# Sliding-window attention inside a fused MLP kernel: two steps at a time, score halves folded into one of 64 keys, a wide softmax over three engines

## The chip, the cores and the metric

One core of a Trainium2 chip runs the kernel. The metric is the device time of one execution in microseconds, as the median of several runs. The core has TensorE (matmul, and the weight loads that precede each), VectorE, ScalarE, GpSimd and SyncE, each with a queue of its own that is worked through in order; semaphores join them. SyncE only issues DMAs.

## The reference, cut to what matters

```python
batch, n_heads, seq, head_dim = (4, 8, 576, 64)
scores = (1 / sqrt(64)) * q @ k.T
mask = (rel >= 0) & (rel < 64)          # rel = query position - key position
scores = where(mask, scores, -1e9)
scores = scores - max(scores)
attn = exp(scores)
attn = attn / (sum(attn) + 1e-9)
x = attn @ v                            # 2304 tokens x 512
h = (x @ w1) * (x @ w2) @ w3 @ w_out    # 512 -> 1024 -> 1024 -> 512
y = x' @ w_in; y = max(0.01 * y, y); y @ w_out2   # 512 -> 2048 -> 512
```

All is float32. The window is 64 keys wide, and queries are taken in blocks of 64, so a block sees two blocks of keys: its own, up to and with the diagonal, and the one before it, above the diagonal. For each query row exactly one of the two halves holds a valid key at a given place, so every row has at most 64 valid keys.

## The kernel before

**Stages.** The products are three passes over high and low parts of float32r (lines 406 to 408), in a seven-product scheme on blocks of 384 tokens. The stages are: the product of the two small weight matrices in 16 slots of 12 matmuls of 512 columns (`wprod_slot`, the early stage); the products of x with w1 and w2 in 168 slots of 6 matmuls of 384 columns (`ab_product`, the order of `AB_SEQ`); and then the later products, which have no part in the change. Attention is laid between the slots of the first two: the first third of it into the early stage, the rest into the second.

**Attention before.** There are 36 steps, each a block of 64 queries of one sequence with all 8 heads, 9 steps to a sequence. Steps go in pairs for the scores and the values. `scores(g)` makes 8 matmuls of 64x64 with 128 keys moving (64 for a step that opens a sequence) into PSUM, two heads on the partitions and four on the free axis. On VectorE `mask_scores` scales and adds the mask in one pass from PSUM to SBUF (L1228) and takes the negated max (L1233). On ScalarE `exps` runs four Exps of 128 columns, each with a bias and an accumulated sum (L841). VectorE adds epsilon and inverts (L1239, L1243), GpSimd multiplies (`normalize`, L771). TensorE turns the 128x128 blocks, four transposes a step (`turn`, L1690), ScalarE copies the turned blocks from PSUM (`turn_copy`, L835), and `values(g)` makes 8 matmuls with 128 rows contracted (L1680). ScalarE or, in the early stage, VectorE copies the values out (`values_copy`, L851, L1248).

**Order.** All is placed by hand, by slots of TensorE. In the early stage the scores of pair p stand behind slot 2p, the turns behind slots 2p+2 and 2p+3, the values behind slot 2p+4. In the second stage the scores stand at slot S (5, 11, 17, 23, 29, 35, 62, 68, 74, 80, 86, 92), the turns in the middle of slots S+8 and S+11, the values at S+12. Each engine runs one loop over the same slots, in which softmax work stands among other work:

- VectorE, early stage, iteration k: values copy, mask passes of what was scored in slot k-1, half of a weight "fill" where `P0_LO` says so (`split_fill`, L1196), the low parts of the pieces for slot k+1 (`split_piece`, L1184), then the sums. Slot k+1 of TensorE waits for these pieces.
- ScalarE: `turn_copy`, the high parts of the pieces, the Exps, fills, and in iteration 7 the copies of two finished banks (`save_wsum`), for which slot 8 waits.
- GpSimd: `normalize`, and the sums of weight quarters (`fill_sums`, four instructions, in iterations 1, 4, 8 and 11 and four times in the second stage; `presums` later).
- In the second stage VectorE makes the sums and products of the seven-product scheme, for which later slots wait with about two slots of slack, and half fills in rounds 1 and 2.

Of the kernel before, what the change touches and what calls it, by code (L numbers as in the profile page):

```python
# [5 lines left out]
F32 = mybir.dt.float32  # L6
F32R = mybir.dt.float32r
ALU = mybir.AluOpType
# [3 lines left out]
P = 128  # L12
# [30 lines left out]
YR0 = AR  # L43
# [32 lines left out]
SCORES0 = tuple(range(CSTEPS))  # L76
TURN0, VALUES0 = 2, 3
SCORES = {}
for _c in range(2):
    for _j in range(CSTEPS):  # L80
        SCORES[(_c + 1) * CSTEPS + _j] = slot_of(4 * _c, 5 + 3 * _j)
EXPS_A, EXPS_B, RECIP, TURN, VALUES = 2, 3, 4, 8, 9


SCORED, VALUED = {}, {}
for _g in range(NSTEP):
    SCORED[_g] = SCORES0[_g - _g % 2] if _g < CSTEPS else SCORES[_g - _g % 2]
    VALUED[_g] = SCORES0[_g | 1] + VALUES0 if _g < CSTEPS else SCORES[_g | 1] + VALUES
# [12 lines left out]
def width(g):  # L101
    return KW if g % NB else BQ
# [113 lines left out]
def build(nc, qk_steps, v_steps, masks, w3, wo, w12, w_in, w_out, out):  # L216
    with ExitStack() as ctx:
# [32 lines left out]
        negmax = sb("negmax", 2 * HP)  # L250
        sums = sb("sums", 2 * HP)
        sums_eps = sb("sums_eps", 2 * HP)
        rsum = sb("rsum", 2 * HP)
# [5 lines left out]
        mask_s = at(2048, 2 * KW).rearrange("p (b k) -> p b k", b=2)  # L259
        v_raw = at(2304, 2 * DM).rearrange("p (r n) -> p r n", r=2)  # L260
        pt = [at(n, HP * P) for n in (3328, 3840, 1536, 4352)]
        probs = [p.rearrange("p (h k) -> p h k", h=HP) for p in pt]
# [31 lines left out]
        ps_more = ctx.enter_context(nc.psum_tensor("ps_more", [P, 512], F32))  # L294
        ps_v = ctx.enter_context(nc.psum_tensor("ps_values", [P, 512], F32))
        ps_turned = ps_more[:, :].rearrange("p (h k) -> p h k", h=HP)
        ps_heads = ps_v[:, :].rearrange("p (h b q) -> p h b q", h=HP, b=2)
# [9 lines left out]
        probs_zero = sem("probs_zero")  # L307
# [5 lines left out]
        masked = sem("masked")  # L313
        max_done = sem("max_done")
        exp_done = sem("exp_done")
        eps_done = sem("eps_done")
# [3 lines left out]
        pt_done = sem("pt_done")  # L320
# [179 lines left out]
        def _(sp):  # L500
# [70 lines left out]
            def load_qk(g):  # L571
                if g >= 2:
                    sp.wait_ge(scores_done, g - 1)
                sp.dma_start(qk[:, g % 2], qk_steps[g]).then_inc(qk_in[g % 2], 16)

            def load_v(g):
                if g >= 2:
                    sp.wait_ge(values_done, g - 1)
                sp.dma_start(v_raw[:, g % 2], v_steps[g]).then_inc(v_in[g % 2], 16)
# [20 lines left out]
            def load_ty(k):  # L600
                if k == 0:
                    sp.wait_ge(values_done, NSTEP)
                    sp.wait_ge(xs_lo, NPROD * NC2)
# [57 lines left out]
            for k in range(WSLOTS):  # L661
                for i in pieces_for(k + 2) if k else ():
                    load_piece(i)
                for g in range(2, CSTEPS + 2):
                    if SCORED[g - 2] == k - 1:
                        load_qk(g)
                    if VALUED[g - 2] == k - 1:
                        load_v(g)
# [11 lines left out]
            for n in range(NSEQ):  # L680
                r = AB_SEQ[n][0]
                m = n - slot_of(r, 0)
                for g in range(CSTEPS + 2, NSTEP):
                    if SCORED[g - 2] == n - 1:
                        load_qk(g)
                    if VALUED[g - 2] == n - 1:
                        load_v(g)
                if r > 0 and m == (4 if slot_of(r, 3) in VALUED.values() else 3):
                    store_p(r - 1)
                    store_p_late(r - 1)  # L690
# [70 lines left out]
        def _(pool):  # L761
# [5 lines left out]
            def normalize(g):  # L767
                r = g % 2
                pool.wait_ge(rsum_done, g + 1)
                w = width(g)  # L770
                pool.tensor_tensor(probs[g % 4][:, :, 0:w], probs[g % 4][:, :, 0:w],  # L771
                                   rsum[:, r * HP:(r + 1) * HP].unsqueeze(2).to_broadcast([P, HP, w]),
                                   ALU.mult).then_inc(probs_done, 1)
# [21 lines left out]
            for k in range(WSLOTS):  # L795
                for g in range(CSTEPS):
                    if SCORES0[g] == k - 1:
                        normalize(g)
                if k in P0_SUMS:
                    fill_sums(P0_SUMS[k])  # L800
            for n in range(NSEQ):
                for g in range(CSTEPS, NSTEP):
                    if SCORES[g] + RECIP == n:
                        normalize(g)
# [8 lines left out]
        def _(act):  # L813
# [19 lines left out]
            def turn_copy(g):  # L833
                act.wait_ge(turned, g + 1)
                act.activation(probs[g % 4], ps_turned, ACT.Copy).then_inc(pt_done, 1)  # L835

            def exps(g, pairs):
                r, w = g % 2, width(g)
                act.wait_ge(max_done, g + 1)
                for u in pairs:  # L840
                    act.activation(probs[g % 4][:, u, 0:w], probs[g % 4][:, u, 0:w], ACT.Exp,  # L841
                                   bias=negmax[:, r * HP + u:r * HP + u + 1], scale=1.0,
                                   accum_out=sums[:, r * HP + u:r * HP + u + 1]).then_inc(exp_done, 1)

            def values_copy(g):
                q, j = g // CSTEPS, g % CSTEPS
                act.wait_ge(values_done, g + 2)
                if j == 0:
                    act.wait_ge(xs_lo, NPROD * q)
                t0 = j % (CSTEPS // 2) * BQ  # L850
# [1105 lines left out]
```

## Time and profile before

| | |
|---|---|
| median of 3 runs | 732.0 us (731.67 to 732.21) |
| span of the profiled execution | 728.8 us |
| TensorE matmul busy | 722.2 us, 99% of the span, 5032 instructions |
| VectorE busy | 530.9 us, 73% |
| ScalarE busy | 416.7 us, 57% |
| GpSimd busy | 101.8 us, 14% |
| granted TensorE clock | 1.000 |
| DMA | 181.13 MB, mean 249 GB/s |

The profiled execution has no time of its own beside its span; the runs lie 2.9 to 3.4 us above it, 3.2 for the median. A busy share near 99% for TensorE says that matmuls follow each other, since their lengths overlap: what counts is the step from one start to the next. In the rows, a start and a length stand first (us), and "idle before" gives what ended a wait.

### The profile page before, as it was taken

The numbers are of one execution on the slowest core, as the hardware profiler recorded it, in microseconds if no ns is written. First come the engines' busy times: TensorE is split into PE (matmuls) and PEld (weight loads), VectorE is DVE, ScalarE is ACT, GpSimd is POOL, SyncE is SP. The second block draws the span as 40 slices with busy tenths as digits, with TensorE's granted clock in tenths as the row PEclk, the third lists the DMA queues.
The fourth block names the chain that finished last, engine by engine and source line by source line (L and its number), as shares of the span: only waits on it lengthen the run. The fifth ranks groups of instructions, "written<-read, shape, count | busy, mean of one in ns | idle before, by whom it ended". The sixth has DMA issues, their size and how long they took to land.

```text
span 728.8 us, 13804 instructions
## 1 busy us (share of the span) xinstructions
PE 722.2 (99%) x5032; PEld 697.9 (96%) x5032; DVE 530.9 (73%) x834; ACT 416.7 (57%) x888; POOL 101.8 (14%) x122
## 2 busy tenths in 40 slices
PE   9999999999999999999999999999999999999998
PEld 7788989999999999999999999999999999999998
DVE  6988888797767679798668968569788655445552
ACT  5876677646664345665555655456677534544541
POOL 3433474413333120000000000000000000000000
PEclk9999999999999999999999999999999999999999
DMA  9884667655754689989857998987996468778773
GB/s 340 291 293 164 206 232 232 200 163 164 244 175 160 195 291 389 324 279 322 289 193 279 318 298 285 364 278 247 381 370 240 128 186 239 206 212 236 208 199 119
DMA packets 96835, 181.13 MB, mean 249 GB/s; under 512 B 7936, under 2 KB 55680, under 8 KB 96768
## 3 DMA queue, kind: packets, MB, share of 16 engines
q1 hardware_dynamic: 90032, 166.62, 69.1%
q10 hardware_dynamic: 6736, 13.63, 5.1%
q8 instruction: 40, 0.66, 0.4%
q14 instruction: 27, 0.22, 0.1%
HBM read 111.80 MB, written 68.42 MB: 247 GB/s over the span
## 4 chain that ended last, share of the span: by engine, by line
PE 61%; DVE 0%; issue 0%; ACT 0%; DVEq 0%
PE acc L406 10%; PE acc L408 9%; PE acc L407 9%; PE ps_pair L406 5%; PE ps_pair L408 5%; PE ps_pair L407 5%; PE ps_more L408 3%; PE ps_values L408 3%; PE ps_more L406 3%; PE ps_values L406 3%; PE ps_more L407 3%; PE ps_values L407 3%; DVE weights_b L1196 0%; DVE arena L1377 0%; DVE arena L1382 0%
## 5 line engine op out<-in xcount | busy, mean ns | idle before, releaser
L406 PE MATMUL acc<-parts,weights_a 128*128 128x384 f32 (+1 forms) x320 | 112.2, 351 | 0.1
L408 PE MATMUL acc<-parts,weights_a 128*128 128x384 f32 (+1 forms) x320 | 109.5, 342 | 0.0
L407 PE MATMUL acc<-parts,weights_a 128*128 128x384 f32 (+1 forms) x320 | 109.3, 341 | 0.0
L406 PE MATMUL acc<-parts,weights_b 128*128 128x384 f32 x320 | 109.1, 341 | 0.2 <-ACT arena L899 0.2
L408 PE MATMUL acc<-parts,weights_b 128*128 128x384 f32 x320 | 107.1, 335 | 0.0
L407 PE MATMUL acc<-parts,weights_b 128*128 128x384 f32 x320 | 107.0, 334 | 0.0
L1462 DVE TENSOR_TENSOR parts<-raw_c,parts 128x768 fp32r<-128x768 f32 x64 | 61.1, 958 | 61.6 <-ACT parts L958 61.5
L958 ACT ACTIVATE parts<-raw_c 128x768 fp32r<-128x768 f32 x64 | 54.0, 846 | 68.9 <-DMA raw_c<-g_between 66.4
L406 PEld LDWEIGHTS acc<-parts,weights_a 128*128 128x128 f32 x320 | 60.1, 188 | 4.6 <-issue 1.7
L841 ACT ACTIVATE arena<-arena,negmax 128x128 f32<-128x128 f32 (+1 forms) x144 | 55.2, 386 | 15.4 <-DVE negmax L1233 15.3
L406 PEld LDWEIGHTS acc<-parts,weights_b 128*128 128x128 f32 x320 | 60.1, 188 | 1.7 <-issue 0.7
L408 PEld LDWEIGHTS acc<-parts,weights_a 128*128 128x128 f32 x320 | 60.1, 188 | 1.7
L407 PEld LDWEIGHTS acc<-parts,weights_a 128*128 128x128 f32 x320 | 60.2, 188 | 1.4
L407 PEld LDWEIGHTS acc<-parts,weights_b 128*128 128x128 f32 x320 | 60.1, 188 | 0.0
L408 PEld LDWEIGHTS acc<-parts,weights_b 128*128 128x128 f32 x320 | 60.1, 188 | 0.0
L937 ACT ACTIVATE arena<-arena 128x384 f32<-128x384 f32 x72 | 35.9, 524 | 41.0 <-DVE arena L1331 18.7
L771 POOL TENSOR_TENSOR arena<-arena,rsum 128x512 f32<-128x512 f32 (+1 forms) x36 | 40.9, 1137 | 100.7 <-DVE rsum L1243 100.7
L912 ACT ACTIVATE parts<-arena 128x768 fp32r<-128x768 f32 x42 | 35.3, 848 | 34.1 <-PE ps_pair L408 10.6
L1403 DVE TENSOR_TENSOR parts<-arena,parts 128x768 fp32r<-128x768 f32 x42 | 39.5, 953 | 13.7 <-ACT parts L912 13.6
L1331 DVE TENSOR_TENSOR arena<-acc,arena 128x384 f32<-128x384 f32 x60 | 31.7, 552 | 17.6 <-PE acc L408 13.1
L406 PE MATMUL ps_pair<-parts,weights_b 128*128 128x384 f32 x120 | 40.2, 335 | 0.0
L407 PE MATMUL ps_pair<-parts,weights_b 128*128 128x384 f32 x120 | 40.1, 334 | 0.0
(213 smaller groups left out, 1764.2 us busy)
## 6 DMA issues: line engine op xcount, KB each, us to landing
g_between<-arena SPq DMA_DIRECT2D x75, 384.0 KB, 4.8
raw_c<-g_between SPq DMA_DIRECT2D x64, 384.0 KB, 3.5
arena<-p_between SPq DMA_DIRECT2D x42, 384.0 KB, 5.2
arena<-qk_steps SPq DMA_DIRECT2D x36, 384.0 KB, 5.0
arena<-v_steps SPq DMA_DIRECT2D x36, 256.0 KB, 3.7
p_between<-arena SPq DMA_DIRECT2D x24, 384.0 KB, 5.9
x_between<-arena ACTq DMA_DIRECT2D x21, 384.0 KB, 5.4
arena<-x_between SPq DMA_DIRECT2D x21, 384.0 KB, 5.2
```

What stands on the lines that cost most here:

```text
L406: eng.matmul(out_ap, w_hi, m_hi, start=start, stop=False, skip_group_check=resumed)
L407: eng.matmul(out_ap, w_hi, m_lo, start=False, stop=False, skip_group_check=resumed)
L408: return eng.matmul(out_ap, w_lo, m_hi, start=False, stop=stop, skip_group_check=resumed)
L771: pool.tensor_tensor(probs[g % 4][:, :, 0:w], probs[g % 4][:, :, 0:w], rsum[:, r * HP:(r + 1) * HP].unsqueeze(2).to_broadcast([P, HP, w]), ...
L841: act.activation(probs[g % 4][:, u, 0:w], probs[g % 4][:, u, 0:w], ACT.Exp, bias=negmax[:, r * HP + u:r * HP + u + 1], scale=1.0, accum_ou ...
L912: act.activation(block_places[k % NPROD][:, 0:BW], ty_raw[TY_SLOT[k]], ACT.Copy).then_inc(ty_hi, 1)
L937: act.activation(g, g, ACT.Prelu, alpha=SLOPE).then_inc(g_done[q], 1)
L958: act.activation(block_places[k % NPROD][:, 0:BW].rearrange("p (j t) -> p j t", j=2), t_source(k), ACT.Copy).then_inc(t_hi, 1)
L1331: dve.tensor_tensor(dest, bank(r, i, s)[:, 0:CT], p1_sb[:, s], ALU.add).then_inc(c11_done, 1)
L1403: dve.tensor_tensor(b[:, BW:2 * BW], ty_raw[TY_SLOT[k]], b[:, 0:BW].bitcast(F32), ALU.subtract).then_inc(ty_lo, 1)
L1462: dve.tensor_tensor(lo, t_source(k), hi.bitcast(F32), ALU.subtract).then_inc(t_lo, 1)
```

## The change

A pair of steps becomes the unit everywhere (18 "duos" in place of 36 steps). The scores stay as they are, except that an opening step writes its own keys to the upper half of its place.

- ScalarE copies the own-keys half of all 16 blocks from PSUM to SBUF (`fold_copy`), 512 columns.
- VectorE overwrites it under a mask with the half of the keys before (`copy_predicated`, once, or twice where a step of the pair opens a sequence), then takes the max over 64 keys, 8 results a partition.
- GpSimd adds the negated max (`shift`); ScalarE runs one Exp of 512 columns with the scale of 1/8 in it; VectorE sums (`tensor_reduce`), adds epsilon, inverts; GpSimd multiplies as before.
- TensorE turns the pair with 4 transposes in place of 8 (`turn`, at 2p+3 and at S+10).
- VectorE writes two masked copies of the turned block from PSUM (`unfold`), one for the keys before and one for the own keys, in place of ScalarE's two copies.
- `values` makes 32 matmuls of 64 rows and 64 columns, two accumulating into each place, in place of 16 of 128 rows; an opening step needs half as many. The results go to two banks.
- The sums and the inversion move one iteration later in the early stage (k-2 for k-1) and to S+5 from S+4 and S+7; the Exps go to S+3, the shift to S+2.

```diff
+            def shift(p):
+                r = p % 2
+                pool.wait_ge(max_done, p + 1)
+                pool.tensor_tensor(probs_flat[r], probs_flat[r],
+                                   negmax[:, r * H:(r + 1) * H].unsqueeze(2).to_broadcast([P, H, BQ]),
+                                   ALU.add).then_inc(shifted, 1)
...
             for k in range(WSLOTS):
...
+                for p in range(CPAIRS):
+                    if SCORED[p] == k - 1:
+                        shift(p)
+                    if SCORED[p] == k - 2:
+                        normalize(p)
                 if k in P0_SUMS:
                     fill_sums(P0_SUMS[k])
...
+            def fold_copy(p):
+                act.wait_ge(scores_done, p + 1)
+                if p >= 2:
+                    act.wait_ge(turned, p - 1)
+                act.activation(probs[p % 2], ps_own, ACT.Copy).then_inc(fold_copied, 1)
+
+            def exps(p):
+                act.wait_ge(shifted, p + 1)
+                act.activation(probs_flat[p % 2], probs_flat[p % 2], ACT.Exp, scale=float(D) ** -0.5).then_inc(exp_done, 1)
...
+            def fold(p):
+                r = p % 2
+                dve.wait_ge(fold_copied, p + 1)
...
+                if whole:
+                    dve.copy_predicated(probs[r], earlier.unsqueeze(1).unsqueeze(1).to_broadcast([P, 2, HP, BQ]),
+                                        ps_before).then_inc(folded, 2)
...
+                dve.tensor_reduce(negmax[:, rr], probs_flat[r], AX.X, ALU.max, negate=True).then_inc(max_done, 1)
+
+            def invert_sums(p):
+                rr = slice(p % 2 * H, (p % 2 + 1) * H)
+                dve.wait_ge(exp_done, p + 1)
+                dve.tensor_reduce(sums[:, rr], probs_flat[p % 2], AX.X, ALU.add).then_inc(sums_done, 1)
...
+            def unfold(p):
+                dve.wait_ge(turned, p + 1)
+                if p > 0:
+                    dve.wait_ge(values_done, p)
+                for c in range(2):
+                    dve.tensor_tensor(pt[c].rearrange("p (u q) -> p u q", q=BQ), ps_more.rearrange("p (u q) -> p u q", q=BQ),
+                                      mask_s[:, 1 + c].unsqueeze(1).to_broadcast([P, H, BQ]), ALU.mult).then_inc(unfolded, 1)
...
+            def values(p):
+                for b in range(2):
+                    pe.wait_ge(v_in[b], 16 * (p + 1))
+                pe.wait_ge(unfolded, 2 * p + 2)
+                pe.wait_ge(x_done, 2 * p)
+                for b in range(2):
+                    for t in range(2):
+                        for c in range(2):
+                            if c == 0 and opens(2 * p + b):
+                                continue
+                            for r in range(2):
+                                for a in range(2):
+                                    d, rows = slice(a * D, (a + 1) * D), slice(r * BQ, (r + 1) * BQ)
+                                    turned_at = ((b * 2 + t) * 2 + (a ^ t)) * BQ
+                                    last = pe.matmul(ps_heads[r][d, t, b], v_raw[rows, b, c, t, a],
+                                                     pt[c][rows, turned_at:turned_at + BQ],
+                                                     start=c == 0 or opens(2 * p + b), stop=c == 1)
+                last.then_inc(values_done, 1)
+
+            def turn(p):
+                pe.wait_ge(probs_done, p + 1)
+                pe.wait_ge(x_done, 2 * p)
+                for n in range(4):
+                    last = pe.transpose(ps_more[:, n * P:(n + 1) * P], probs[p % 2][:, n // 2, n % 2 * 2:n % 2 * 2 + 2], ident[:, :])
+                last.then_inc(turned, 1)
```

## Rows read from the trace of the kernel before

**Rows 1.** The page's busy line: us, share of the span, instructions.
```profile
PE 722.2 (99%) x5032; PEld 697.9 (96%) x5032; DVE 530.9 (73%) x834; ACT 416.7 (57%) x888; POOL 101.8 (14%) x122
```

**Rows 2.** TensorE's waits: us in total, times, longest.
```profile
PE ps_more L1690 <- POOL arena L771: 1.5, 1, 1.5
```

**Rows 3.** Windows: length, busy us of each engine (x instructions), clock, DMA.
```profile
5.00:70.00 65.00, 64.82 (x628) 52.03 (x628) 54.89 (x93) 48.04 (x145) 26.01 (x28) 1.00 0.78 276
76.00:108.00 32.00, 30.33 (x333) 28.16 (x333) 27.49 (x48) 21.87 (x71) 21.56 (x21) 1.00 0.66 216
```

**Rows 4.** Timeline of TensorE around one turn: start, length, instruction.
```profile
86.38 0.60 PE L1690 MATMUL ps_more<-ident,arena 128*128 128x128 f32 x4
86.73 0.42 PE L406 MATMUL acc<-weights_a 128*128 128x384 f32 x1
86.99 0.34 PE L407 MATMUL acc<-weights_a 128*128 128x384 f32 x1
87.16 0.34 PE L408 MATMUL acc<-weights_a 128*128 128x384 f32 x1
```

**Rows 5.** TensorE: values of a pair, then 64-wide scores; lengths of scores (ns).
```profile
103.44 1.15 PE L1680 MATMUL ps_values<-arena 128*64 128x64 f32 x32
...
104.52 0.46 PE L1700 MATMUL ps_pair<-arena 64*64 64x64 f32 x16
...
L1700 PE MATMUL ps_pair<-arena x576: 216/269/321, 8.3 to 203.6; 64*64 64x128 f32 x168, 64*64 64x64 f32 x24
```

**Rows 6.** Softmax instructions by form: count, busy us, mean ns, idle before.
```profile
L1233 DVE TENSOR_REDUCE negmax<-arena 128x4 f32<-128x512 f32 x32 | 22.0, 686 | 1.1
L1228 DVE SCALAR_TENSOR_TENSOR arena<-ps_pair,arena 128x512 f32<-128x512 f32 x32 | 21.7, 679 | 0.9 <-PE ps_pair L1700 0.7
L1239 DVE TENSOR_SCALAR sums_eps<-sums 128x4 f32<-128x4 f32 x36 | 7.2, 199 | 1.8 <-ACT arena L841 1.5
L841 ACT ACTIVATE arena<-arena,negmax 128x128 f32<-128x128 f32 x128 | 49.8, 392 | 13.6 <-DVE negmax L1233 13.5
L835 ACT ACTIVATE arena<-ps_more 128x512 f32<-128x512 f32 x36 | 21.4, 595 | 27.9 <-PE ps_more L1690 27.9
L771 POOL TENSOR_TENSOR arena<-arena,rsum 128x512 f32<-128x512 f32 x32 | 38.2, 1195 | 85.1 <-DVE rsum L1243 85.1
```

**Rows 7.** Timeline of VectorE: a mask pass and its max.
```profile
34.00 0.69 DVE L1228 SCALAR_TENSOR_TENSOR arena<-ps_pair,arena 128x512 f32<-128x512 f32 x1 [0.16 <-PE ps_pair L1700]
34.72 0.69 DVE L1233 TENSOR_REDUCE negmax<-arena 128x4 f32<-128x512 f32 x1
```

**Rows 8.** Timeline of VectorE: the same fill split twice.
```profile
17.57 1.18 DVE L1196 TENSOR_TENSOR weights_a<-raw_a,weights_a 128x768 fp32r<-128x768 f32 x1
...
30.80 0.95 DVE L1196 TENSOR_TENSOR weights_a<-raw_a,weights_a 128x768 fp32r<-128x768 f32 x1
```

**Rows 9.** Timeline of GpSimd: two normalises, first and last sum of a fill.
```profile
16.89 1.04 POOL L771 TENSOR_TENSOR arena<-arena,rsum 128x512 f32<-128x512 f32 x1
...
25.44 0.74 POOL L778 TENSOR_TENSOR raw_a<-raw_a 128x256 f32<-128x256 f32 x1
...
28.27 1.06 POOL L783 TENSOR_TENSOR raw_a<-raw_a 128x256 f32<-128x256 f32 x1
29.65 1.04 POOL L771 TENSOR_TENSOR arena<-arena,rsum 128x512 f32<-128x512 f32 x1 [0.32 <-DVE rsum L1243]
```

**Rows 10.** Timeline of TensorE: first matmuls of slots 4, 8 and 12.
```profile
20.00 0.50 PE L406 MATMUL acc<-parts,weights_a 128*128 128x512 f32 x1
...
37.84 0.47 PE L406 MATMUL acc<-parts 128*128 128x512 f32 x1
...
54.97 0.48 PE L406 MATMUL acc<-parts,weights_a 128*128 128x512 f32 x1
```

**Rows 11.** Timeline of VectorE: fill splits of the second stage.
```profile
94.52 1.80 DVE L1196 TENSOR_TENSOR weights_b<-raw_b,weights_b 128x768 fp32r<-128x768 f32 x1
...
98.78 3.27 DVE L1196 TENSOR_TENSOR weights_b<-raw_b,weights_b 128x1024 fp32r<-128x1024 f32 x2
```

More of the change, by code:

```diff
@@ L682, in _ @@
                 m = n - slot_of(r, 0)
[L683 to L688, printed above, removed]
+                for p in range(CPAIRS, NDUO - 1):
+                    if SCORED[p] == n - 1:
+                        load_qk(2 * p + 2)
+                        load_qk(2 * p + 3)
+                    if VALUED[p] == n - 1:
+                        load_v(2 * p + 2)
+                        load_v(2 * p + 3)
+                if r > 0 and m == (4 if slot_of(r, 3) in LATE_VALUED else 3):
                     store_p(r - 1)
@@ L801, in _ @@
             for n in range(NSEQ):
[L802 to L804 removed]
+                for p in range(CPAIRS, NDUO):
+                    if SCORED[p] + EXPS_A == n:
+                        shift(p)
+                    if SCORED[p] + RECIP == n:
+                        normalize(p)
                 if n in AB_SUMS:
@@ L1469, in _ @@
             for k in range(WSLOTS - 1):
-                for g in range(CSTEPS):
-                    if g % 2 == 0 and VALUED[g] == k - 1:
-                        values_copy(g)
-                for g in range(CSTEPS):
-                    if SCORES0[g] == k - 1:
-                        mask_scores(g)
+                for p in range(CPAIRS):
+                    if VALUED[p] == k - 1:
+                        values_copy(p)
+                for p in range(CPAIRS):
+                    if TURNED[p] == k - 1:
+                        unfold(p)
+                    if SCORED[p] == k - 1:
+                        fold(p)
                 if k in P0_LO:
@@ new lines, in turn, with scores @@
+            def turn(p):
[3 more added lines that the diff above has]
+                    last = pe.transpose(ps_more[:, n * P:(n + 1) * P], probs[p % 2][:, n // 2, n % 2 * 2:n % 2 * 2 + 2], ident[:, :])
+                last.then_inc(turned, 1)
+            def scores(p):
+                for b in range(2):
+                    pe.wait_ge(qk_in[b], 16 * (p + 1))
+                pe.wait_ge(folded, 2 * p)
+                for b in range(2):
+                    k0 = BQ if opens(2 * p + b) else 0
+                    for h in (0, 1, 4, 5, 2, 3, 6, 7):
+                        u, half = h // 2, h % 2
+                        place = half ^ (h >= H // 2)
+                        d, x = slice(half * D, (half + 1) * D), slice(place * BQ, (place + 1) * BQ)
+                        last = pe.matmul(ps_scores[b][x, u, k0:KW], qk[d, b, h // 2 * BQ:(h // 2 + 1) * BQ],
+                                         qk[d, b, QN + u * KW + k0:QN + (u + 1) * KW], start=True, stop=True)
@@ new lines, in attention_first @@
+                for p in range(CPAIRS):
+                    if SCORED[p] == k:
+                        scores(p)
+                for p in range(CPAIRS):
+                    if TURNED[p] == k:
+                        turn(p)
+            def attention(n):
+                for p in range(CPAIRS, NDUO):
+                    if VALUED[p] == n:
+                        values(p)
+                for p in range(CPAIRS, NDUO):
+                    if SCORED[p] == n:
+                        scores(p)
@@ L1789, in turns @@
             def turns(k):
-                for g in range(CSTEPS, NSTEP):
-                    if SCORES[g] + TURN == k:
-                        turn(g)
+                for p in range(CPAIRS, NDUO):
+                    if TURNED[p] == k:
+                        turn(p)
             def ab_product(k, r, i, s):
```

287 lines of the change are left out of this document (114 added, 173 removed).

## The prediction, made before the changed kernel was run

> **What bounds the kernel now.** I read the page first, then the waits of TensorE, then the timelines of the two stages that hold attention, engine by engine. TensorE is busy 722.2 us of a span of 728.8 [rows 1], and almost nothing holds it: the largest wait is 1.5 us, once, for GpSimd [rows 2]. So a TensorE instruction taken away counts in full, and so does every new wait, while work of the other engines is free as long as it is in time. How near they are to being late is seen in the windows: up to 70 us VectorE is busy 54.9 of 65 us, between 76 and 108 us 27.5 of 32 and GpSimd 21.6 [rows 3]. Attention ends near 222 us; after it nothing changes.
>
> **TensorE, what goes.** Of 8 transposes in a pair of steps 4 remain. A turn of 4 costs more than its 0.35 us: the next start is 0.35 later and the one behind it 0.26 instead of 0.17, so 0.44 us in all [rows 4]. Twelve late pairs save 5.3 us; six early ones, whose dropped turn stood right behind the scores and shared their switch, 0.39 each by the same reading, 2.3. The wait of 1.5 us for GpSimd goes too, with 0.2 us of slower transposes (its turn moves to 10 slots after the scores). Gross gain 9.3 us.
>
> **TensorE, what comes.** The values grow from 16 matmuls of 128 rows to 32 of 64x64 (24 where a step opens a sequence). Each matmul leaves 2 records, so 32 become 64. The rows of the same shape are the 64-wide scores: 16 records of 8 matmuls fill 0.46 us, of which 0.22 is the last one's own length [rows 5]; so starts are about 16 ns apart, against 30 for the values of now (1.15 less 0.22, 31 starts [rows 5]). 64 records at 15 to 16 ns are 0.95 us: no change for a full pair, 0.2 less for the four that open, which is why I take 0 to -0.8 in total. From above, if quadrants did not run together, 64 at 30 ns are 1.9 us, 0.95 more, some 15 us for all. The new order walks all four quadrants, as the scores do, so I take the first. The Trainium skill (TensorE: Matmul & The Clock Gate, Part 1, the section on 56 against 53.3 ns) says that matmul starts never come closer than about 25 ns. By that 64 records would be an estimated 1.6 us and the change 10 us worse than I sum. The scores' starts, 16 ns apart, are against it; it is one form of rival (c).
>
> **The other engines, prices.** The predicated copy is not in the trace: not under 0.61 us (the step between plain 512-wide instructions), not over the 1.19 of GpSimd's 512-wide one; I take 0.68, the 512-wide instruction from PSUM with a mask that it replaces, and with the wait behind it 0.72 to the reduce [rows 6, 7]. Fold copy 0.60, a max or sum reduce 0.69 (0.61 to the next start), shift like normalise, 1.04 undisturbed, wide Exp 0.60 by ScalarE's 512-wide copy, unfold twice 0.68 [rows 6]. ScalarE gains: 8 Exps of 0.39 and 2 copies, 4.3 us a pair, become 1.2. VectorE per pair: 2x1.37 and four small ones of 0.2 = 3.5 become 0.68 + 2x0.69 + 2x0.2 + 2x0.68 = 3.8. These sums say little: what counts is order. Before, the mask pass starts as soon as the scores are readable. Now VectorE stands behind ScalarE's copy, ScalarE's Exp behind GpSimd's shift, and each engine's queue holds weight splitting for the next slot of TensorE behind the wait.
>
> **Sharing between VectorE and GpSimd.** A split with two SBUF inputs slows when GpSimd works: at 17.57 the 768-wide one takes 1.18, where GpSimd's normalise runs until 17.93, and 0.95 at 30.80, after the normalise of 29.65 has ended [rows 8, 9]. The Trainium skill (SBUF — State Buffer, Who interferes with whom) calls this an exclusive lock on a shared port pair; the rows agree. Before, the normalise follows the reciprocal, and VectorE then goes to a mask pass, which has one input in PSUM and keeps its 0.68. Now the shift is released by the max, just when VectorE turns to its splits: they alternate, and the second split comes a shift (1.0) late.
>
> **Early stage, slot by slot.** R is when scores are readable. TensorE can start the next even slot at R - 0.1 + 2.77 (12 matmuls 0.23 apart) + 0.44 (turn) = R + 3.1 (2.7 for slot 2, which has no turn). VectorE has the max at R + 0.6 + 0.72 + 0.61 = R + 1.95; then splits.
> Slot 2: fold in two halves, splits 2x0.61, shift between: R + 4.3, wait 1.6.
> Slot 4: a fill split of 0.87 first: 1.95 + 0.87 + 1.22 + 1.0 = R + 5.0, wait 1.9.
> Slot 6: GpSimd's four weight sums, 3.9 us from 25.44 to 29.33 [rows 9], are queued ahead of the shift and alternate with the splits: R + 3.9, wait 0.9. The shift comes only after them, at R + 4.6, and ScalarE, which stands in Exp, reaches the pieces of slot 7 over 7 us after R. VectorE waits for that at its fill: slot 7 waits 0.3 and VectorE enters the next fold 1.8 late.
> Slot 8: needs ScalarE's copy of the first bank, which stands behind the Exp. Before, slot 8 began at 37.84 [rows 10]. Now R + 1.75 (VectorE late) + 1.3 + 0.65 (piece) + 1.04 + 0.6 + 0.6 = R + 5.9; TensorE is ready at R + 3.4: wait 2.5.
> Slot 12: 1.95 + fill 1.13 + shift 1.04 + piece 0.7 = R + 4.9, wait 1.8.
> Sum 9.0 us of new waits. Against it: turns 2.3, waits of today that are in these (0.3 at slot 4, 0.35 at slot 8 and small ones, 0.8 together), and opening values 0.4. Net +5.5 (bounds: +1.9 if shift and splits never meet, +8 with the dear predicated copy).
>
> **Middle stage, 76 to 150 us.** VectorE has a backlog: fills of 1.80 and 3.27 (two) between 94.52 and 102 beside GpSimd's sums [rows 11]. The old values did not depend on VectorE; ScalarE copied the turned block. The unfold now does, and stands behind these fills. From the same start of the fills (the queue ahead is equal: two mask passes out, one unfold and two sum reduces in), 94.1 + 1.8 + 0.5 + 1.3 + 0.5 + 3.3 + 1.3 = 102.8 for the unfold of the eighth pair, while TensorE reaches its values at 100.3: wait 2.5. The same reckoning gives 1.5 for the ninth pair, then about none. Turns -2.65, old wait -1.7, new waits +4.0, opening values -0.2: net -0.5 (bounds -4.5 and +3).
>
> **Last stage, 156 to 222 us.** No fills. Turns -2.65, opening values -0.2. Three unfolds sit behind a product that ends with their slot, 2.0 us against 2.1 allowed: 0.1 each. One Exp waits for a shift behind GpSimd's 2.6 us of sums and delays a bank copy: 0.25. Net -2.3.
>
> DMAs move with their pairs, of equal size and slots; SP's queue issues value loads a pair at a time, behind the same products. Scores keep their widths.
>
> **Sum.** +5.5 - 0.5 - 2.3 = +2.7 on a span of 728.8: 731.5. The median of the runs, 732.0, lies 3.2 above the span; so 734.7.
>
> **Rivals.** (a) Splits and shift do not meet, or VectorE's piece always gets in first: early stage +1.9, total -0.9, 731.1. For it: one split is often already running when the shift is released; against: rows 8. Chance 0.20.
> (b) The other side, faster: queues run ahead of my chains. Today VectorE is as full and TensorE waits nowhere; if ScalarE's 3.1 us saved per pair lets weight pieces and fills be split earlier, only slots 4, 8 and 12 wait, for 4.5 us together, and the middle stage about 0.5: 732.0 - 9.3 - 0.8 + 5 = 727. It decides if the splits of slot 2 and 6 are ready on time. Against: in order queues put the pieces behind the fold. Chance 0.23.
> (c) The quadrants of the values do not run together, in whole or by half (two matmuls now add into one place, which the scores never do): 64 records at 22 to 30 ns instead of 15, +8 to +15, 742 to 749. Chance 0.07.
> (d) The predicated copy is near 1.19, or the backlog of the middle stage reaches more pairs: +3 to +5, 738. Chance 0.10.
> The forecast itself, 732.3 to 737: 0.40.
>
> **Numbers.** About 0.2% (1.5 us) is what a measurement can tell. Slower: 0.40 less a little, plus (c), (d): 0.55. Within: (a) and edges, 0.22. Faster: 0.23. The range of 8 in 10 goes from inside (b), 728.5, to over (d), 740; the likeliest case alone is 732.3 to 737.
>
> **What would show it.** The values x64 records in about 1.15 us; starts of slots 4, 8 and 12 late by about 3, 5 and 6 us against 20.00, 37.84 and 54.97; splits of 1.2 instead of 0.68 behind the shift; the end of the early stage about 5.5 late; TensorE's waits for VectorE at two groups of values near 100 to 115 us; no wait at the turn near 101. Wrong would be: values over 1.5 us, slot 8 before 40, or no wait at all at the unfolds.

## The result, and the profile after

The changed kernel takes 737.3 us (736.9 to 740.0), the kernel before in the same session 732.1; ratio 1.0083, interval [1.0066, 1.0101]. Slower, as forecast; 2.6 over the forecast of 734.7 and inside its range. The profiled execution took 737.4 with a span of 735.6. The forecast was 731.5 for the span, so by the profile it is 4.1 short: the time lies 1.8 above the span here, while the 3.2 that the forecast added holds for the kernel before's median against its one profile.

The page of the changed kernel, busy line (against [rows 1]), and its table of TensorE's waits (against [rows 2]):

```profile
PE 714.7 (97%) x5472; PEld 689.8 (94%) x5472; DVE 537.1 (73%) x819; ACT 363.4 (49%) x600; POOL 102.7 (14%) x122
```

```profile
PE ps_values L1716 <- DVE arena L1268: 5.8, 5, 2.5
PE acc L408 <- DVE parts L1195: 4.1, 3, 1.8
PE acc L408 <- ACT arena L873: 1.6, 1, 1.6
PE ps_values L1922 <- POOL ident L771: 1.5, 1, 1.5
PE acc L408 <- DVE weights_a L1195: 1.4, 1, 1.4
PE acc L408 <- DVE arena L1367: 1.4, 1, 1.4
PE ps_pair L408 <- ACT arena L914: 0.7, 1, 0.7
PE acc L408 <- ACT arena L919: 0.6, 1, 0.6
```

TensorE is 7.5 us less busy, and waits that were not there stand against it: for VectorE's unfolds (L1268), for its splits of weight pieces (L1195) and for ScalarE's bank copy (L873). The last three lines lie behind attention. The windows, those of [rows 3] first:

```profile
5.00:70.00 65.00, 57.78 (x680) 45.24 (x680) 53.22 (x82) 28.33 (x46) 30.00 (x28) 0.97 0.78 265
76.00:108.00 32.00, 29.52 (x306) 27.83 (x305) 29.20 (x43) 14.58 (x25) 17.83 (x17) 1.00 0.63 208
...
20.00:25.00 5.00, 3.21 (x13) 2.40 (x12) 5.00 (x7) 2.62 (x4) 1.69 (x1) 0.82 0.83 275
25.00:30.00 5.00, 5.00 (x91) 3.90 (x91) 3.16 (x7) 0.58 (x2) 2.31 (x3) 0.84 0.58 185
```

ScalarE has fallen from 48 to 28 us in the first window, VectorE and the span of the stage have not. The granted clock is below 1.00, which the forecast had not thought of. TensorE's timeline shows where (slots 4, 8 and 12 against [rows 10]):

```profile
20.62 0.60 PE L1725 MATMUL ps_values<-ident,arena 128*128 128x128 f32 x4
23.02 0.63 PE L408 MATMUL acc<-parts,weights_a 128*128 128x512 f32 x1 [1.79 <-DVE parts L1195]
23.44 0.63 PE L409 MATMUL acc<-parts,weights_a 128*128 128x512 f32 x1
...
26.43 0.50 PE L410 MATMUL acc<-parts,weights_a 128*128 128x512 f32 x1
26.76 0.39 PE L408 MATMUL acc<-parts,weights_a 128*128 128x512 f32 x1
...
36.68 1.16 PE L1716 MATMUL ps_values<-arena 64*64 64x64 f32 x64
...
43.75 0.47 PE L408 MATMUL acc<-parts 128*128 128x512 f32 x1 [1.61 <-ACT arena L873]
...
61.59 0.50 PE L408 MATMUL acc<-parts,weights_a 128*128 128x512 f32 x1 [1.45 <-DVE weights_a L1195]
...
81.87 1.10 PE L1738 MATMUL ps_pair<-arena 64*64 64x128 f32 x32
...
223.05 1.16 PE L1716 MATMUL ps_values<-arena 64*64 64x64 f32 x64
```

Behind the wait of 1.79 eight matmuls are 0.43 apart and not 0.23: TensorE ran at 1.2 GHz, half of its 2.4, from 23.0 to 26.4 (a "half clock" below), and these eight took 8 x 0.20 = 1.6 us longer. The scores of pair 6, the first after the early stage, begin at 81.9 (before: 76.0), the last values at 223.1 (before: 219.6), and 512.5 us follow (before: 509.2).

VectorE and GpSimd around slot 4, where the forecast had the two take turns:

```profile
19.96 0.95 DVE L1207 TENSOR_TENSOR weights_a<-raw_a,weights_a 128x768 fp32r<-128x768 f32 x1
20.83 1.53 DVE L1195 TENSOR_TENSOR weights_a<-arena,weights_a 128x512 fp32r<-128x512 f32 x1
22.28 0.68 DVE L1195 TENSOR_TENSOR parts<-arena,parts 128x512 fp32r<-128x512 f32 x1
```

```profile
20.12 1.69 POOL L777 TENSOR_TENSOR arena<-arena,negmax 128x512 f32<-128x512 f32 x1 [1.53 <-DVE negmax L1250]
```

A split of 0.68 takes 1.53 while the shift works, and the shift, 1.04 alone, takes 1.69. Prices of the new instructions, by form:

```profile
L777 POOL TENSOR_TENSOR arena<-arena,negmax 128x512 f32<-128x512 f32 x18 | 24.8, 1377 | 52.4 <-DVE negmax L1250 52.4
L1250 DVE TENSOR_REDUCE negmax<-arena 128x8 f32<-128x512 f32 x18 | 12.4, 687 | 0.6
L858 ACT ACTIVATE arena<-arena 128x512 f32<-128x512 f32 x18 | 11.4, 631 | 34.6 <-POOL arena L777 34.5
L1239 DVE COPY_PREDICATED arena<-arena,ps_pair 128x512 f32<-128x512 int32 x14 | 10.5, 746 | 5.0 <-ACT arena L854 5.0
```

The third line is the one to remember: ScalarE works 11.4 us in its 18 wide Exps and stands 34.5 us in front of them, waiting for GpSimd's shift; 15.1 us of that are in front of the six Exps of the early stage.

### The profile page after: what moved, and what is told of

Read it like the earlier page. It is cut to its first block, busy times and chain, and to the rows that moved or that the text cites. A ratio compares the mean times of both kernels' runs of the same rounds, so it can differ in the third digit from the quotient of the medians.

```text
span 735.6 us, 14358 instructions
## 1 busy us (share of the span) xinstructions
PE 714.7 (97%) x5472; PEld 689.8 (94%) x5472; DVE 537.1 (73%) x819; ACT 363.4 (49%) x600; POOL 102.7 (14%) x122
## 4 chain that ended last, share of the span: by engine, by line
PE 56%; DMA 2%; ACT 1%; issue 1%; DVE 1%; ACTq 0%; DVEq 0%; SPq 0%
PE acc L408 8%; PE acc L409 8%; PE acc L410 8%; PE ps_values L409 5%; PE ps_values L410 5%; PE ps_values L408 5%; PE ps_pair L408 5%; PE ps_pair L409 5%; PE ps_pair L410 5%; DMA x_between<-arena 1%; DMA p_between<-arena 1%; DMA arena<-p_between 0%; ACT weights_a L848 0%; ACT arena L946 0%; DVE arena L1357 0%
## 5 line engine op out<-in xcount | busy, mean ns | idle before, releaser
L927 ACT ACTIVATE parts<-arena 128x768 fp32r<-128x768 f32 x42 | 35.3, 848 | 35.0 <-PE ps_pair L410 10.9
L1429 DVE TENSOR_TENSOR parts<-arena,parts 128x768 fp32r<-128x768 f32 x42 | 39.6, 954 | 14.5 <-ACT parts L927 14.4
L410 PE MATMUL ps_values<-parts,weights_b 128*128 128x384 f32 x132 | 44.1, 334 | 0.0
L408 PE MATMUL ps_values<-parts,weights_b 128*128 128x384 f32 x132 | 44.1, 334 | 0.0
L409 PE MATMUL ps_values<-parts,weights_b 128*128 128x384 f32 x132 | 44.1, 334 | 0.0
L408 PE MATMUL ps_pair<-parts,weights_b 128*128 128x384 f32 x120 | 40.2, 335 | 0.7 <-ACT arena L914 0.7
```

The lines of the kernel that those rows point to most:

```text
L408: eng.matmul(out_ap, w_hi, m_hi, start=start, stop=False, skip_group_check=resumed)
L409: eng.matmul(out_ap, w_hi, m_lo, start=False, stop=False, skip_group_check=resumed)
L410: return eng.matmul(out_ap, w_lo, m_hi, start=False, stop=stop, skip_group_check=resumed)
L927: act.activation(block_places[k % NPROD][:, 0:BW], ty_raw[TY_SLOT[k]], ACT.Copy).then_inc(ty_hi, 1)
L1429: dve.tensor_tensor(b[:, BW:2 * BW], ty_raw[TY_SLOT[k]], b[:, 0:BW].bitcast(F32), ALU.subtract).then_inc(ty_lo, 1)
```

## The experiments

Unless it is said otherwise, each edits the changed kernel. A time is a median, the ratio is to the kernel before in the same session, and square brackets behind a time hold its interval. The last three columns come from each kernel's one profile: the start of the scores of pair 6 (pairs are counted from 0; this is the end of the early stage), from there to the start of the last values, and what is left of the span.

| kernel | time, us | ratio to before | pair 6 | to last values | rest |
|---|---|---|---|---|---|
| before | 732.1 | | 76.0 | 143.6 | 509.2 |
| changed | 737.3 | 1.0083 | 81.9 | 141.2 | 512.5 |
| e7_same_again | 737.4 | 1.0069 | 82.2 | 143.7 | 510.8 |
| e1_pieces_first | 746.7 | 1.0211 | 92.9 | 141.7 | 510.1 |
| e2_no_shift | 729.4 | 0.9971 | 77.5 | 138.1 | 511.9 |
| e3_unfold_first | 737.3 | 1.0096 | 82.1 | 143.8 | 509.5 |
| e4_fill_wait | 735.3 | 1.0060 | 81.7 | 143.1 | 509.1 |
| e5_bias_exps | 732.5 | 1.0010 | 80.5 | 139.0 | 511.3 |
| e6_unfold_early | 734.3 | 1.0042 | 82.1 | 139.6 | 511.9 |
| e8_pieces_before_fold | 737.4 | 1.0097 | 82.1 | 143.7 | 509.6 |
| e9_combined | 736.1 | 1.0055 | 83.9 | 140.8 | 509.6 |
| e10_combined_bias | 731.2 | 0.9997 | 81.6 | 138.5 | 510.3 |
| e11_exp_later | 731.5 | 1.0004 | 75.1 | 142.2 | 509.6 |
| e12_two_softmaxes | 727.0 | 0.9936 | 75.1 | 138.8 | 509.1 |

The profiles of the last two are of the fastest of their executions (728.6 and 724.8), 2.9 and 2.2 us under their medians, so their columns flatter them by so much.

**Pieces ahead of everything** (`e1_pieces_first`).

```diff
             for k in range(WSLOTS - 1):          # VectorE
+                for i in pieces_for(k + 1):
+                    split_piece(i)
...
-                for i in pieces_for(k + 1):
-                    split_piece(i)
```

(and on ScalarE ahead of `fold_copy`)

> In the early stage VectorE and ScalarE split the pieces of slot k+1 ahead of the fold, not behind it. If the new waits are a matter of order in the queues, the four waits of TensorE for splits (1.35 at slot 2, 1.79 at slot 4, 0.99 at slot 6, 1.45 at slot 12) go, and with the wait at slot 4 the half clock behind it (8 matmuls 0.43 apart and not 0.23, 1.6 us); the wait of 1.6 for ScalarE at slot 8 stays. That is 7.2 us less: about 730. The rival is that VectorE is simply full (53.2 of 65 us): then the folds and the inversions come later, the waits turn up at the early turns or values in place of slots 2 to 12, and the time is 735 to 738.

Measured: 746.7, [1.0195, 1.0226]. The four waits went (0.72 came at slot 3), but TensorE waited 4.84, 1.81, 3.77 and 2.29 us for unfolds, with half clock behind three of the four. Why, VectorE's timeline shows:

```profile
25.43 1.29 DVE L1195 TENSOR_TENSOR parts<-arena,parts 128x512 fp32r<-128x512 f32 x2 [3.06 <-ACT parts L836]
26.64 1.28 DVE L1268 TENSOR_TENSOR arena<-ps_values,arena 128x512 f32<-128x512 f32 x2
```

```profile
23.30 0.63 ACT L858 ACTIVATE arena<-arena 128x512 f32<-128x512 f32 x1 [5.06 <-POOL arena L777]
23.83 1.04 ACT L848 ACTIVATE weights_a<-raw_a 128x1024 fp32r<-128x1024 f32 x1
24.78 1.13 ACT L836 ACTIVATE parts<-arena 128x512 fp32r<-128x512 f32 x2
```

The unfold stands behind the low parts, these wait for ScalarE's high parts, and ScalarE stood 5.06 us in front of the Exp. Neither theory had named this queue.

**No shift** (`e2_no_shift`).

```diff
-                        shift(p)                 # GpSimd, both loops
...
-                act.wait_ge(shifted, p + 1)
+                act.wait_ge(max_done, p + 1)
```

> The subtraction of the max is left out: GpSimd's shift is gone and the Exp takes the unshifted scores once the max is made (the quotient is the same as long as nothing overflows). If splits and shift hold each other up, the splits that stand beside a shift fall from 1.53 to 0.68 and from 2.13 for two to 1.28; each of the waits at slots 2, 4, 6 and 12 shrinks by 0.85 and the one at slot 8 by the shift's 1.4: 7.2 us of early waits become about 2.4, the half clock behind slot 4 may go too (1.6), and the time is 730 to 732.5. The rival is that only the place behind the fold counts and the shift costs the splits nothing: then only slot 8 gains, 1.4, and the time is about 736.

Measured: 729.4, [0.9962, 0.9981], below the kernel before, but without the subtraction of the max. The split at slot 4 takes 0.69 again. The waits at slots 2, 4, 6 and 12 are 1.03, 0.94, 0.69 and 0.98 (before the edit 1.35, 1.79, 0.99 and 1.45), slot 8 waits not at all: 7.2 us of waits become 4.0 (with one of 0.34 at slot 10) and not the 2.4 expected, so the sharing was worth less than expected. No half clock is left, and the second stage is 3 us shorter too. The shift as a whole costs 7.9 us; how much of it is sharing and how much the longer chain, this run does not separate.

**Unfold at the head of its iteration** (`e3_unfold_first`).

```diff
             for n, (r, i, s) in enumerate(AB_SEQ):
+                for p in range(CPAIRS, NDUO):
+                    if TURNED[p] == n:
+                        unfold(p)
                 if i == P1:
                     make_c11(r, s)
```

> In the second stage VectorE makes the unfold at the head of the iteration of its slot, ahead of the sums of the seven-product scheme. If the unfold is late because of what stands ahead of it, the waits at the values (2.48, 0.33, 1.50 and 1.25 us at 100.1, 109.4, 119.6 and 179.4) shrink to under 1 us together, and the time is 732 to 733.5. The rival is a backlog that has to be worked off anyway: the sums are then late in place of the unfold, TensorE waits for them, and the time stays at 736.5 to 738.

Measured: 737.3, [1.0074, 1.0118], the values' waits nearly the same (2.48, 0.64, 1.18 and 1.25, and 0.68 at 199.8). The unfold overtook next to nothing: VectorE was about two slots behind, so what delayed it stood in earlier iterations. The run decides nothing between place and backlog.

**The wait at slot 4 filled** (`e4_fill_wait`).

```diff
+                if k == 4:
+                    for _ in range(8):
+                        pe.matmul(ps_v[:, 0:P], ident[:, :], ident[:, :], start=True, stop=True)
                 wprod_slot(k)
```

> Eight matmuls of the 128x128 identity, whose results nothing reads, stand ahead of slot 4 and fill its wait of 1.79 us. If the half clock of 23.0 to 26.4 follows from TensorE's standing still before it, slot 4 still starts at 23.0 to 23.3, its twelve matmuls are 0.23 apart and the granted clock of 20 to 30 us is 1.00 instead of 0.82 and 0.84; slot 5 starts 1.3 to 1.6 earlier than at 29.28 and the time is about 736. The rival is that the low clock comes from something else (a time since the start, the load of the other engines): it stays at 23 to 26.4 and the time at 737 to 738.

Measured: 735.3, [1.0045, 1.0075], 2 us less than the changed kernel, though its two intervals, [1.0066, 1.0101] and [1.0052, 1.0086], overlap with this one. In the early stage the profile is 0.8 to 1.4 shorter (from the first scores to those of pair 6 72.5, against 73.3 and 73.9 in the two profiles of the changed kernel). Timeline and windows (the whole run began 0.7 later, so slot 4 starts at the same distance from the first scores):

```profile
21.75 1.95 PE L1926 MATMUL ps_values<-ident 128*128 128x128 f32 x16
23.70 0.50 PE L408 MATMUL acc<-parts,weights_a 128*128 128x512 f32 x1
```

```profile
20.00:25.00 5.00, 5.00 (x33) 4.28 (x32) 4.97 (x8) 2.67 (x5) 1.69 (x1) 1.00 0.82 271
25.00:30.00 5.00, 5.00 (x95) 4.00 (x94) 4.50 (x8) 1.63 (x4) 1.70 (x2) 1.00 0.82 280
100.00:105.00 5.00, 5.00 (x105) 4.77 (x106) 2.62 (x7) 1.20 (x2) 3.66 (x4) 0.67 0.35 112
```

At slot 4 the clock stays full, and the slot starts no later. That the filler did it is not shown: in three further profiles, `e3_unfold_first`, `e6_unfold_early` and `e7_same_again`, the clock also stays full at slot 4, behind the same wait with nothing in it. The line of `e7_same_again`, whose length is 0.50 and not 0.63:

```profile
22.77 0.50 PE L408 MATMUL acc<-parts,weights_a 128*128 128x512 f32 x1 [1.79 <-DVE parts L1195]
```

At 100 us, behind the wait of 2.48 for the unfold, the clock falls in this run, where in the changed kernel's profile it did not.

**Exps with a bias in place of shift, wide Exp and sum** (`e5_bias_exps`).

```diff
+                act.activation(bias[:, b:b + H], negmax[:, b:b + H], ACT.Copy, scale=float(D) ** -0.5)
+                for u in range(H):
+                    act.activation(probs_flat[p % 2][:, u], probs_flat[p % 2][:, u], ACT.Exp,
+                                   bias=bias[:, b + u:b + u + 1], scale=float(D) ** -0.5,
+                                   accum_out=sums[:, b + u:b + u + 1]).then_inc(exp_done, 1)
```

> The wide softmax alone is undone, the folding stays: no shift on GpSimd and no sum on VectorE; ScalarE scales the negated max (one small instruction, about 0.2) and runs eight Exps of 64 columns with a bias and an accumulated sum (a 128-wide one took 0.39, so 0.33 to 0.39 each, 2.7 to 3.1 a pair in place of 0.6). If the early waits come from the shift that stands beside the splits, they shrink as without a shift, and VectorE is another 0.67 a pair freer: 728 to 731. The rival is that ScalarE becomes the late one: its pieces of the next slot and the bank copies of slot 8 stand behind 2.9 us of Exps, the waits at slots 4, 8 and 12 stay or grow, and the time is 734 to 738.

Measured: 732.5, [1.0001, 1.0020], between the two forecasts. Both were half right: the second stage gains 2 to 5 us, and in the early stage the wait at slot 4 shrinks to 0.94, but slot 8 waits 2.47 for ScalarE.

**Unfold two iterations earlier for pairs 6, 7, 8 and 12** (`e6_unfold_early`).

```diff
+UNFOLDED = {_p: TURNED[_p] - (2 if _p in (6, 7, 8, 12) else 0) for _p in range(CPAIRS, NDUO)}
-                    if TURNED[p] == n:
+                    if UNFOLDED[p] == n:
                         unfold(p)
```

> For the four pairs whose values waited (pairs 6, 7, 8 and 12) VectorE's unfold stands two iterations earlier, ahead of the sums of the products and of the fills that it stood behind; moving it to the head of its own iteration changed nothing, since VectorE ran about two slots behind. If the place is the cause, the waits of 2.48, 0.33, 1.50 and 1.25 at the values go down to under 1 us together and the time is 731.5 to 733.5. The rival is a backlog: VectorE is so full between 85 and 122 us that the sums and fills, now behind, make TensorE wait by the same amount, 736 to 738.

Measured: 734.3, [1.0027, 1.0057]. The values' waits fall from 5.8 to 0.9, and 2.6 us of new waits for VectorE's sums (L1359 there, `make_c11`) appear at 102.9 and 125.9. So about half of it was the place, and about half VectorE's backlog.

**No edit** (`e7_same_again`).

> The changed kernel with no edit, for a second profile. Behind the end of attention it took 3.3 us longer than the kernel before (512.5 against 509.2 from the last values), in three waits at 277.7, 309.5 and 394.4; the other kernels took 509.1 to 512.0 there. If this stretch is slower because of the change, the three waits stand in the same places again; if it is the chance of how the DMAs fall, the stretch takes another time between 509 and 512.5 and other waits. And the half clock: if it belongs to the wait at slot 4 it stands there again, at 23.0; if it may follow any wait of over about 2 us, it is found at another wait, as at 100 us in e4_fill_wait.

Measured: 737.4, [1.0052, 1.0086]. The rest behind the last values takes 510.8 with waits at other places; over all kernels here, which all end alike, it is 509.1 to 512.5. So most of the 3.3 us that this part added in the first profile is not the change's, and the kernel before had nearly the lowest value. The half clock is not at slot 4 here, whose wait is the same 1.79, but behind slot 8's wait and again behind that of the values at 100:

```profile
40.00:45.00 5.00, 2.73 (x10) 2.05 (x9) 5.00 (x8) 2.12 (x4) 1.28 (x1) 0.83 0.99 361
45.00:50.00 5.00, 5.00 (x107) 4.01 (x106) 1.56 (x6) 1.03 (x2) 3.88 (x5) 0.82 0.64 197
100.00:105.00 5.00, 4.61 (x102) 4.31 (x103) 2.90 (x7) 1.19 (x2) 3.20 (x4) 0.66 0.45 124
```

**Pieces ahead of the fold alone** (`e8_pieces_before_fold`).

```diff
+                scored = any(SCORED[p] == k - 1 for p in range(CPAIRS))
+                if scored:
+                    for i in pieces_for(k + 1):
+                        split_piece(i)
                 ...  # fold
-                for i in pieces_for(k + 1):
+                for i in () if scored else pieces_for(k + 1):
```

(and on ScalarE ahead of `fold_copy`, as in `e1_pieces_first`)

> As e1_pieces_first, but VectorE splits the pieces ahead of the fold alone: in the iterations with an unfold they stay behind it, where in the first try they held it up and the values waited 1.5 to 5 us each. ScalarE has its pieces ahead of the fold copy. If the order is what costs in the early stage, the waits at slots 2, 4, 6 and 12 (5.6 us in the second profile of the changed kernel too) go, the one at slot 8 stays, one half clock of 1.7 may go with them, and the time is 730 to 732. The rival is that the fold, 1.3 later, makes the turn or the unfold late in place of the slot: waits at the early turns and values of about the same sum, 735 or more.

Measured: 737.4, [1.0069, 1.0125]. Slots 2 and 4 no longer wait and slot 6 only 0.35, but slots 3, 5, 7 and 13 do, 0.81, 1.77, 1.74 and 1.43, and slot 8 2.99; pair 6 begins at 82.1, as without the edit, though no half clock falls into the stage this time. Moving the pieces ahead of the fold moves the waits and takes nothing away.

**Three moves together**, on the wide softmax (`e9_combined`) and on the one with a bias (`e10_combined_bias`): the order of the last run, the unfold two earlier for pairs 6 and 12, and `save_wsum` ahead of `exps` in iteration 7.

> The order of e8_pieces_before_fold, the unfold two iterations earlier for pairs 6 and 12 alone (where it took nothing from the sums that TensorE needs), and in iteration 7 ScalarE's two bank copies ahead of the Exp. If waits are all that eats the gain, about 5.6 (slots 2 to 12), 2 (slot 8), 3.5 (values of pairs 6 and 12) and one or two stretches of half clock of 1.7 go: 725 to 728, under the kernel before. The rival, VectorE full in the early stage and to 125 us: the waits come up elsewhere and the time is 731 to 734.

> The same three moves on the kernel with eight Exps with a bias in place of the shift, the wide Exp and the sum. VectorE and GpSimd have 2 us a pair less to do, ScalarE 2.3 more. If the sharing of VectorE and GpSimd still costs after the moves (the fills of 3.3 for two and the sums beside GpSimd's between 95 and 125 us), this one is 1 to 3 us under e9_combined: 723 to 727. If the order was all, it is equal to it within 1 us, or over it where ScalarE's Exps delay the pieces of the next slot.

Measured: 736.1, [1.0036, 1.0075], and 731.2, [0.9987, 1.0007]. Both missed. In `e9_combined` the wait at slot 8 fell from 2.99 to 0.55, but pair 6 began at 83.9, 1.8 later than before the moves: waits of 1.00 and 2.09 came up at later slots, and a half clock behind the second. The one with a bias is 4.9 under it, more than the 1 to 3 expected.

**The Exp one iteration later** (`e11_exp_later`). The edit of `e8_pieces_before_fold`, and on ScalarE:

```diff
                 for p in range(CPAIRS):
-                    if SCORED[p] == k - 1:
+                    if SCORED[p] == k - 2:
                         exps(p)
```

> The order of e8_pieces_before_fold, and in the early stage ScalarE's Exp one iteration later, behind the pieces of the next slot. Until now the scores of pair 6 began at 82.1 us whatever was moved in VectorE's queue or filled on TensorE; only without the shift they began at 77.5. So what sets the early stage is thought to be one chain through in-order queues: the pieces of the next slots stand on ScalarE behind the Exp, which stands behind GpSimd's shift, which stands behind VectorE's max. If that is right, the pieces come loose from the chain, the waits at slots 5, 7, 8, 9 and 12 go, scores of pair 6 begin at 76 to 78, and the time is 730 to 733. If VectorE or the DMAs of the pieces are full in this stage (the rival), they still begin at 81 to 82.5 and the time is 736 to 738.

Measured: 731.5, [0.9990, 1.0018], 5.9 us less than with the order alone; the Exp's move without that order was not run. TensorE's timeline of this kernel:

```profile
32.88 0.50 PE L408 MATMUL acc<-parts,weights_a 128*128 128x512 f32 x1 [0.15 <-DVE parts L1195]
37.56 0.50 PE L408 MATMUL acc<-parts 128*128 128x512 f32 x1 [0.54 <-DVE arena L1284]
57.98 0.50 PE L408 MATMUL acc<-parts,weights_a 128*128 128x512 f32 x1 [1.17 <-DVE weights_a L1195]
61.81 0.50 PE L408 MATMUL acc<-parts 128*128 128x512 f32 x1 [0.37 <-DVE parts L1195]
75.06 1.10 PE L1743 MATMUL ps_pair<-arena 64*64 64x128 f32 x32
```

Of the changed kernel's 7.2 us of early waits 2.2 are left, with VectorE doing the same work. Pair 6 begins 7.0 earlier than without the edit and 1.0 earlier than in the kernel before.

**Wide softmax early, Exps with a bias late** (`e12_two_softmaxes`). The same order; `exps` as in `e5_bias_exps` for `p >= CPAIRS`.

> The wide softmax in the early stage, in the order of e11_exp_later (scores of pair 6 began at 75.1), and in the second stage the eight Exps with a bias of e5_bias_exps, where ScalarE has room and VectorE and GpSimd do not (from the scores of pair 6 to the last values it took 139.0 us with them, 142.2 with the shift in e11_exp_later, 143.6 in the kernel before). If the two parts add, the last values begin at 213.5 to 215, and with 509 to 512 behind them the span is 724 to 727 and the time 726 to 729, below the kernel before (731.3 to 732) by 0.4 to 0.8%. If the clock falls behind the waits that are left, up to 1.7 more; if they don't add, because the early gain is taken back by VectorE's backlog at 95 us, 730 to 732.

Measured: 727.0, [0.9920, 0.9952], the one version here that beats the kernel before with nothing left out. Its table of waits, and the scores of pair 6 and the last values in its timeline:

```profile
PE acc L410 <- ACT arena L906: 2.6, 2, 1.3
PE ps_values L1734 <- DVE arena L1281: 1.6, 2, 1.3
```

```profile
75.11 1.10 PE L1756 MATMUL ps_pair<-arena 64*64 64x128 f32 x32
...
213.94 1.16 PE L1734 MATMUL ps_values<-arena 64*64 64x64 f32 x64
```

The parts add: 75.1 and 138.8, as the two parents have them. Its six runs show a granted clock of 1.000, where the changed kernel's eight show 0.995 or 0.998.

## Why the prediction was right, and where it was not

- **Gross gain.** Held, as far as it can be worked back from waits. Up to the last values the changed kernel is 3.4 us late, with 12.9 us of waits there (5.8 + 4.1 + 1.6 + 1.4) and 1.6 of half clock: the gain is 14.5 - 3.4 = 11.1. Forecast: 9.3, 0.8 of waits today and 0.8 of opening values, 10.9. `e11_exp_later`, at full clock, gives nearly the same: 9.2 of waits and 2.4 earlier, 11.6.
- **Values.** Held. 64 records take 1.16 [rows 5: 1.15 for 32], 48 take 0.93; rival (c) is out. From the first start to the last are 1.16 - 0.22 = 0.94 us, 15 ns a record, 30 ns a matmul. The Trainium skill's 25 ns between starts (TensorE: Matmul & The Clock Gate, Part 1) is contradicted only if it is read by the record, as the prediction did; by the matmul the trace agrees.
- **Prices.** Predicated copy 0.75 for 0.68 taken, Exp 0.63 for 0.60, shift 1.38 on average for 1.04 undisturbed, the others to 0.02. Rival (d)'s 1.19 is out.
- **VectorE beside GpSimd.** Held and larger: 1.53 where 1.2 was forecast.
- **Early waits.** 1.35, 1.79, 0.99, 1.61 and 1.45 at slots 2, 4, 6, 8 and 12 for 1.6, 1.9, 0.9, 2.5 and 1.8; slots 4, 8 and 12 late by 3.0, 5.9 and 6.6 for 3, 5 and 6; the stage late by 5.8 for 5.5. That the stage fits so well is partly luck: the waits sum to 7.2 where 9.0 was forecast, and a half clock of 1.6, not forecast, fills most of the gap. But the reason given for slots 2 to 6 and 12, pieces behind the fold on VectorE, doesn't carry the stage: `e8_pieces_before_fold` takes it away and gains nothing. What carries it is a chain that the prediction gives for slots 7 and 8 alone: ScalarE's pieces behind its Exp, behind the shift, behind the max (`e11_exp_later`).
- **Middle and last stage.** From pair 6 to the values of pair 11 -0.6 for -0.5 forecast; in the last stage -1.8 for -2.3, with a wait of 1.25 at 179.4 that was not forecast. The middle's sum held, its places did not: the forecast had no wait at pair 6, 2.5 at pair 7 (its "eighth pair") and 1.5 at pair 8, 4.0 in all; measured are 2.48, 0.33 and 1.50, 4.3 in all. The large one is not behind the fills. Pair 6's unfold stands behind sums and products of the seven-product scheme, beside GpSimd's weight sums, and the fills come only after it, taking 0.95 and 2.62 where the prediction kept 1.80 and 3.27:

```profile
97.58 1.07 DVE L1409 TENSOR_TENSOR arena<-arena 128x384 f32<-128x384 f32 x1
98.58 1.27 DVE L1268 TENSOR_TENSOR arena<-ps_values,arena 128x512 f32<-128x512 f32 x2
...
101.28 0.95 DVE L1207 TENSOR_TENSOR weights_b<-raw_b,weights_b 128x768 fp32r<-128x768 f32 x1
```

- **The term left out** is the clock: the sum lets a wait cost its length. Behind waits of 1.8 us and more TensorE is at times granted half its clock, for about 3.4 us each time in the changed kernel's profiles, which costs 1.6 to 1.7 (in `e1_pieces_first`, behind the wait of 4.84, the stretch is twice as long). Half a clock for 3.4 of 736 us is a mean of 0.998, which three of the changed kernel's four runs show, one showing 0.995; the kernel before shows 0.999 or 1.000 in every run that lists it. Within one kernel, of the eight runs of `e6_unfold_early` the one at 1.000 took 732.6, the four at 0.998 734.1 on average, the three at 0.995 735.8; the five of `e9_combined` go the same way, 733.9, 735.4 and 736.3, while in `e10_combined_bias` and `e11_exp_later` runs at full clock are as slow as some at 0.998. One or two such stretches are 1.7 to 3.4 us, and the forecast was short by 2.6. That they are the whole of it is argued and not shown: the loss in the early stage is in part made up by shorter waits behind it (slot 8 waits 1.61 behind the half clock at slot 4, and 2.27 where it did not fall there).
- **"After it nothing changes"** held for the work. The rest varies by 3.4 us from profile to profile, which the forecast's range should have held a share for. In the spans of the two profiles it is most of the miss: of the 4.1 us over the forecast, 3.3 are in the rest and 0.8 up to the last values. In the second profile of the changed kernel, with two half clocks, the share turns round: 1.6 in the rest, 3.6 up to the last values.

## What to carry to other kernels

Follow a new step through every in-order queue that it passes, and ask on each engine what stands behind the instruction that waits: here ScalarE stood 15.1 us in front of six Exps of 0.63 and held up weight pieces that had nothing to do with the softmax, and moving the Exp behind them brought 5.9 us. Where a wait only moves when the order in one queue is changed, the chain runs through another queue. A step moved to GpSimd can cost VectorE too (0.68 became 1.53 here), and a wait of TensorE of 1.8 us was at times followed by a loss of 1.6 more.

## What the runs showed of the hardware

- The half clock follows a wait, but not each one: the same 1.8 us at slot 4 brought it in one of four profiles, the same 2.5 us ahead of the values of pair 6 in four of seven. There it made the values and scores behind it almost twice as long, as in `e3_unfold_first` (1.16 and 1.10 elsewhere):

```profile
100.36 1.97 PE L1717 MATMUL ps_values<-arena 64*64 64x64 f32 x64 [2.48 <-DVE arena L1268]
102.04 1.97 PE L1739 MATMUL ps_pair<-arena 64*64 64x128 f32 x32
```

- 8 matmuls whose results nobody reads, put in a wait of 1.8 us, delayed nothing. Whether they keep the clock up is open, since it stayed up behind that wait in three of four profiles without them.
- Of six waits of 2.2 to 3.0 us at slot 8, three were followed by half clock (2.27, 2.27 and 2.26) and three were not (2.27, 2.47 and 2.99), so the length of the wait does not decide it.
- An Exp of 64 columns with an accumulated sum takes 0.336 us and starts 0.33 after the one before, so eight of them are 2.7 us against 0.63 for one of 512 columns.
